# Splitting the second layer's weights piece by piece during the first layer, with a detour through DRAM

## What is computed

```python
def _attn_ref(x, filt_r, filt_i):
    X = np.fft.rfft(x, axis=1)
    F = (filt_r + 1j * filt_i)[None, :, :]
    return np.fft.irfft(X * F, n=x.shape[1], axis=1).astype(np.float32)

def _moe_ref(x, w_in, w_out):                 # first layer
    h = x @ w_in
    g = np.where(h > 0.0, h, np.exp(np.minimum(h, 0.0)) - 1.0)
    return g @ w_out

def _moe2_ref(x, w_in, w_out):                # second layer
    h = x @ w_in
    g = h * np.clip(h + 3.0, 0.0, 6.0) / 6.0
    return g @ w_out
```

## Time and profile before

| | us |
|---|---|
| median of 3 runs | 1116.21 (1115.38 to 1118.57) |
| the profiled execution's own time | 1117.79 |
| its span in the profile | 1116.0 |
| PE busy | 1101.5 (99%) |
| ACT busy | 769.0 (69%) |
| DVE busy | 751.9 (67%) |
| POOL busy | 280.7 (25%) |
| TensorE's mean granted clock | 0.998 of full |

### The profile page before, as it was taken

The page is one execution under the profiler, slowest core; times in us unless marked ns, Lnnn a source line. Parts: engine busy times, 40 slices in busy tenths (PEclk is TensorE's granted clock), DMA queues, the critical chain, the costliest instruction groups (busy, mean ns, idle before and its releaser), DMA issues.

```text
span 1116.0 us, 13377 instructions
## 1 busy us (share of the span) xinstructions
PE 1101.5 (99%) x4796; PEld 882.5 (79%) x4796; DVE 751.9 (67%) x933; ACT 769.0 (69%) x1156; POOL 280.7 (25%) x217
## 2 busy tenths in 40 slices
PE   8999999999999999999999999999999999999998
PEld 4565788888888888888888788888888888888886
DVE  5898566666667666666687866666666665665655
ACT  0445588888788888888899766665666566666654
POOL 3856402102102111111288821111111121120000
PEclk9999999999999999999999999999999999999999
DMA  9665300200200200200311200200101001000000
GB/s 283 195 196 177 132 1 1 75 1 1 74 1 1 75 1 1 75 1 1 112 38 57 93 1 1 75 1 15 61 1 37 37 1 38 37 1 1 38 1 37
DMA packets 29618, 54.98 MB, mean 49 GB/s; under 512 B 3440, under 2 KB 19696, under 8 KB 29552
## 3 DMA queue, kind: packets, MB, share of 16 engines
q1 hardware_dynamic: 22784, 42.98, 11.8%
q10 hardware_dynamic: 6768, 11.16, 2.9%
HBM read 35.61 MB, written 18.51 MB: 48 GB/s over the span
## 4 chain that ended last, share of the span: by engine, by line
PE 85%; ACT 4%; DVE 3%; DMA 3%; POOL 2%; issue 2%; SPq 0%; ACTq 0%; DVEq 0%; POOLq 0%
PE ps L471 43%; PE ps L462 13%; PE ps L461 13%; PE ps L460 13%; DMA w_raw<-w_dev 2%; PE ps L424 2%; DVE e L779 1%; ACT e L626 1%; PE ps L394 1%; ACT e L628 1%; ACT w_hi L598 1%; PE ps L402 1%; DMA x_ring<-x_dev 1%; POOL f_ring L824 1%; PE ps L411 1%
## 5 line engine op out<-in xcount | busy, mean ns | idle before, releaser
L793 DVE TENSOR_TENSOR g_lo<-e,g_hi 128x502 fp32r<-128x502 f32 (+1 forms) x288 | 277.2, 990 | 136.1 <-ACT g_hi L665 135.9
L460 PE MATMUL ps<-op_hi,w_hi 128*128 128x502 f32 x672 | 261.9, 390 | 1.6 <-ACT ps L658 1.6
L462 PE MATMUL ps<-op_lo,w_hi 128*128 128x502 f32 x672 | 261.9, 390 | 0.0
L461 PE MATMUL ps<-op_hi,w_lo 128*128 128x502 f32 x672 | 261.2, 389 | 0.0
L471 PE MATMUL ps<-g_lo,w_hi 128*128 128x502 f32 x766 | 236.8, 390 | 0.8 <-DVE g_lo L793 0.6
L471 PE MATMUL ps<-g_hi,w_hi 128*128 128x502 f32 x766 | 235.6, 389 | 0.0
L471 PE MATMUL ps<-g_hi,w_lo 128*128 128x502 f32 x766 | 234.9, 388 | 0.0
L862 POOL TENSOR_TENSOR op_lo<-op_raw,op_hi 128x1004 fp32r<-128x1004 f32 (+1 forms) x48 | 100.3, 2089 | 488.8 <-ACT op_hi L606 488.8
L471 PEld LDWEIGHTS ps<-g_lo,w_hi 128*128 128x128 f32 x766 | 143.3, 188 | 31.8 <-DVE g_lo L793 3.2
L471 PEld LDWEIGHTS ps<-g_hi,w_lo 128*128 128x128 f32 x766 | 144.1, 188 | 29.3
L471 PEld LDWEIGHTS ps<-g_hi,w_hi 128*128 128x128 f32 x766 | 143.8, 188 | 29.4 <-ACT g_hi L665 0.5
(11 more groups left out here) (73 smaller groups left out, 1154.3 us busy)
## 6 DMA issues: line engine op xcount, KB each, us to landing
op_raw<-y SPq DMA_DIRECT2D x36, 251.0 KB, 3.6
x_ring<-x_dev SPq DMA_DIRECT2D x32, 192.0 KB, 4.6
y<-ystage SPq DMA_DIRECT2D x12, 502.0 KB, 2.9
y<-ystage ACTq DMA_DIRECT2D x24, 235.0 KB, 2.8
out_dev<-ystage SPq DMA_DIRECT2D x11, 502.0 KB, 2.9
f_ring<-f_dev SPq DMA_DIRECT2D x13, 384.0 KB, 3.8
w_raw<-w_dev ACTq DMA_DIRECT2D x16, 256.0 KB, 4.3
w_raw<-w_dev SPq DMA_DIRECT2D x16, 256.0 KB, 3.0
```

The costliest lines, as they stand in the source:

```text
L460: pe.matmul(out, w_hi[p][:, cols], hi, start=start, stop=False, skip_group_check=True)
L461: pe.matmul(out, w_lo[p][:, cols], hi, start=False, stop=False, skip_group_check=True)
L462: pe.matmul(out, w_hi[p][:, cols], lo, start=False, stop=True, skip_group_check=True).then_inc(done, 1)
L793: return dve.tensor_tensor(g_lo[:, tiles, :], e[:, tiles, :], f32(g_hi[:, tiles, :]), ALU.subtract)
```

## The change

The second layer's eight pairs are no longer split at the change of layers, but in super-tiles 1 to 4, two pairs in each: `next_weights(s)` gives pairs 2s - 2 and 2s - 1. Their high and low parts are made in a new SBUF buffer, `w_out`, and stored to a DRAM tensor, `w1_parts`. In super-tile 5, as soon as `d12_done` says that a pair's place is free, SP loads both parts (720,896 bytes each) straight into `w_hi[p]` and `w_lo[p]`.

```diff
+        w1_parts = nc.dram_tensor("w1_parts", (PAIRS, 2, P, WCOL), F32, kind="Internal").ap()
+        w_out = sbuf(ctx, "w_out", [P, 2, WCOL], F32R)
+        def next_weights(s):
+
+            return (2 * s - 2, 2 * s - 1) if 1 <= s <= PAIRS // 2 else ()
...
                 if s:
                     store_out(s - 1, 0)
                     store_out(s - 1, 1)
+                for p in next_weights(s):
+                    load_w(PAIRS + p)
+                for p in next_weights(s):
+                    sp.wait_ge(w_hi_done, PAIRS + p + 1)
+                    sp.dma_start(w1_parts[p, 0], f32(w_out[:, 0, :])).then_inc(w1_hi_stored, 16)
+                    sp.wait_ge(w_lo_done, PAIRS + p + 1)
+                    sp.dma_start(w1_parts[p, 1], f32(w_out[:, 1, :])).then_inc(w1_lo_stored, 16)
                 if s == NS - 1:
+                    sp.wait_ge(w1_hi_stored, 16 * PAIRS)
+                    sp.wait_ge(w1_lo_stored, 16 * PAIRS)
                     for p in range(PAIRS):
-                        load_w(PAIRS + p)
+                        sp.wait_ge(d12_done, (NS - 1) * PAIRS + p + 1)
+                        sp.dma_start(f32(w_hi[p][:]), w1_parts[p, 0]).then_inc(w1_loaded[p], 16)
+                        sp.dma_start(f32(w_lo[p][:]), w1_parts[p, 1]).then_inc(w1_loaded[p], 16)
...
-                    if s % NS == 0:
-                        pe.wait_ge(w_hi_done, s // NS * PAIRS + p + 1)
-                        pe.wait_ge(w_lo_done, s // NS * PAIRS + p + 1)
+                    if s == 0:
+                        pe.wait_ge(w_hi_done, p + 1)
+                        pe.wait_ge(w_lo_done, p + 1)
+                    if s == NS:
+                        pe.wait_ge(w1_loaded[p], 32)
...
-                k = u - 2 - (NS - 1) * PAIRS
-                if 0 <= k < PAIRS:
-                    weight_hi(PAIRS + k)
+                if u < NU and p in (1, PAIRS - 1) and next_weights(s):
+                    weight_hi(PAIRS + next_weights(s)[p // (PAIRS - 1)])
...
-                if s != NS - 1:
-                    for piece in range(NOP if s + 1 < 2 * NS else 0):
-                        operand_lo(s + 1, piece)
-                else:
-                    for k in range(PAIRS):
-                        weight_sums(PAIRS + k)
-                        if 1 <= k <= NOP:
-                            operand_lo(s + 1, k - 1)
-                        weight_lo(PAIRS + k)
+                later = next_weights(s)
+                if later:
+                    weight_sums(PAIRS + later[0])
+                    weight_lo(PAIRS + later[0])
+                for piece in range(NOP if s + 1 < 2 * NS else 0):
+                    operand_lo(s + 1, piece)
+                if later:
+                    weight_sums(PAIRS + later[1])
+                    weight_lo(PAIRS + later[1])
```

More of the change, by code:

```diff
@@ L212, in build @@
         w_sum, w_hi_done, w_lo_done = sem("w_sum"), sem("w_hi_done"), sem("w_lo_done")
+        w1_hi_stored, w1_lo_stored = sem("w1_hi_stored"), sem("w1_lo_stored")
+        w1_loaded = [sem(f"w1_loaded{p}") for p in range(PAIRS)]
         xr_loaded, t_sum = sem("xr_loaded"), sem("t_sum")
@@ L593, in weight_hi @@
             def weight_hi(k):
-                p = k % PAIRS
-                if k >= PAIRS:
-                    act.wait_ge(d12_done, (NS - 1) * PAIRS + p + 1)
+                dst = w_hi[k][:] if k < PAIRS else w_out[:, 0, :]
+                if k > PAIRS:
+                    act.wait_ge(w1_hi_stored, 16 * (k - PAIRS))
+                    act.wait_ge(w_lo_done, k)
                 act.wait_ge(w_sum, 4 * (k + 1))
-                act.copy(w_hi[p][:], w_raw[:, k % 2, P:12 * P]).then_inc(w_hi_done, 1)
+                act.copy(dst, w_raw[:, k % 2, P:12 * P]).then_inc(w_hi_done, 1)
             def operand_hi(s, piece):
@@ L838, in weight_lo @@
             def weight_lo(k):
-                p = k % PAIRS
+                hi, lo = (w_hi[k], w_lo[k]) if k < PAIRS else (w_out[:, 0], w_out[:, 1])
                 pool.wait_ge(w_hi_done, k + 1)
+                if k > PAIRS:
+                    pool.wait_ge(w1_lo_stored, 16 * (k - PAIRS))
                 half = WCOL // 2
[L842 to L845, removed]
+                pool.tensor_tensor(lo[:, 0:half], w_raw[:, k % 2, P:P + half],
+                                   f32(hi[:, 0:half]), ALU.subtract)
+                pool.tensor_tensor(lo[:, half:], w_raw[:, k % 2, P + half:],
+                                   f32(hi[:, half:]), ALU.subtract).then_inc(w_lo_done, 1)
             def operand_sums(s):
```

## The result

| | before | changed kernel |
|---|---|---|
| median, us | 1117.32 (6 runs, 1115.38 to 1118.57) | 1129.37 (6 runs, 1127.09 to 1131.79) |
| span of the profiled execution, us | 1116.0 | 1130.0 |
| the profiled execution's own time, us | 1117.79 | 1131.79 |

The change made the kernel slower by 12 us: the ratio is 1.0106, with a 95% interval of 1.0092 to 1.0121. The changed kernel's runs lie in two groups of three, near 1131 (mean granted clock 0.994 to 0.995 of full) and near 1127.5 (0.996 to 0.998). The profiled execution is of the upper one; a second trace, whose time is that of the lower one, comes with the experiments.

A forecast was written before the change was run, and what follows sets the result against it. PE, busy 99%, was taken to bound the kernel. Waits 20.4, second pair 0.8 and later evacuation 1.8, less 2.5 gained, made 20.5 us more; on the median of 1116.21 the forecast was 1136.7, range 1129 to 1144.

The forecast's parts named there:

- lower bounds: Low end of the sum: four super-tiles at 4.0 us less the 2.5 gained, 13.5 us more, 1129.7.
- What bounds the kernel, and what there was to gain: PE, busy 99%; across the change of layers, removing the splitting of weights gains at most 2.5 us.
- The place of the wait: ACT's weight_hi at p = 1 would wait for POOL's sums of the first pair, in four super-tiles.
- The length of the wait: ACT would stand still 4.9 us at p = 1, making PE's p6 4.0 us late.
- From ACT's wait to p6: 4.42 us from weight_hi's start to the next copy's start, and 0.57 for the copy, before PE's p6.
- The second wait, for g_hi and g_lo: PE's g_lo matmuls in the next iteration would be 5.0 us late, against 4.0 at p6; POOL's low parts hinder DVE.
- The clock rival: TensorE's clock falls in the four new waits, costing 0.7 to 1.7 us each: 1139.5 to 1143.5; chance 32%.
- The second pair at p = 7: Its weight_hi fills ACT's idle time before the evacuation: 0.2 us of PE at each of four boundaries, 0.8.
- The later evacuation: ACT's evacuation some 0.6 us later delays the next group's sums: 0.6 us in super-tiles 2, 3 and 4, so 1.8.
- The stores and the reload: 16 DMAs storing the parts and 16 loads bringing them back, 720,896 bytes each, would cost nothing.
- loads land sooner: Rival: raw weights land at the median 3.1 us, each wait costs 1.7, 6.9 us more: 1123.1; chance 12%.

The follow-up runs named there:

- other pair first: The changed kernel with the two pairs' raw loads in the other order, so the pair needed at p = 1 is loaded second: 1134.99 us.
- the tokens' loads first: The changed kernel with the first pair's weight_hi at p = 2 and the second pair's stores behind the next tokens' loads: 1115.03 and 1115.44 us.
- low part later: The changed kernel with POOL's weight_lo of the first pair moved behind the first operand_lo, weight_hi still at p = 1: 1123.35 us.

## Why the prediction was right, and where its numbers were off

The forecast was 1136.7 us in a range of 1129 to 1144, slower with 95%. The time was 1129.37: the sign and the mechanism were right, the size was not. The forecast increase was 20.5 us, the measured one 12.1, three fifths of it and less than the 13.5 of the lower bounds. That the time lies 0.4 us inside the range is luck: the kernel before came out at 1117.32 over six runs, and on the 1116.21 from which the forecast started the same increase would have given 1128.3.

- **What bounds the kernel, and what there was to gain.** Right. 2.5 us were read from the eight intervals, and 2.48 came; by the second trace of the kernel before it is 1.6.
- **The place of the wait.** Right: ACT at p = 1, four times, for POOL's last sum, in the order of the earlier trace rows.
- **The length of the wait.** This is the step that failed. The prediction put ACT's wait at 4.9 us, and with it 4.0 us before p6 in each super-tile; measured are waits of 2.2 to 2.9 us in one trace and 1.7 to 2.5 in the other, and excesses of 1.8 to 2.6 and 1.3 to 2.1 us. Of the 20.4 us in the sum 16 were this term, and it measured 8.8 and 6.5. "The trace shows this very chain at super-tile 5" took the landing there, 6.5 us, for that of any super-tile. In super-tile 1 it was 224.15 - 219.52 = 4.6. The sums took 2.3 us where they had taken 2.8, and the issue came 0.2 later after ACT's evacuation. 4.9 - 1.9 - 0.5 + 0.2 = 2.7. The row that should have raised a doubt was used for a rival only: a median landing of 3.1. One landing behind other transfers is one value out of a range, here 3.8 to 6.5 us.
- **From ACT's wait to p6.** Right to 0.1 us in super-tile 1: `weight_hi` started at 226.46, and 226.46 + 4.42 + 0.57 = 231.45, PE's p6 at 231.51.
- **The second wait, for g_hi and g_lo.** 1.0 us each was forecast. 0.96 to 1.03 was measured in each of the five cases in which the clock did not fall in these two traces, and moving `weight_lo` took it away. The cause given, DVE's operation beside `weight_lo`, holds together with ACT's lateness, not alone.
- **The clock rival.** It came true in part: three falls in one trace, none behind the waits in the other. The price written was 0.7 to 1.7 each. In the changed kernel it was 0.4 to 0.7 (1.66, 1.63 and 1.41 against 0.96), with the other pair first 0.7 to 1.2. The waits were also shorter than the 4.0 us for which it was weighed.
- **The second pair at p = 7.** 0.8 us were put at the boundaries, and 0.3 came, nearly all of it from u = 41. With the tokens' loads first it was 0, so it is not `weight_hi` at p = 7 that costs it, but the order of tokens and stores on SP, which the prediction had put at nothing.
- **The later evacuation.** 1.8 us were added for it. The evacuation does come later behind p6, 8.6 us in place of 8.2 in super-tiles 2 to 4, but the second raw load is issued 10.49 to 10.53 us behind p6 there and 10.33 in super-tile 1, so that 0.2 us of it are left. No such term is seen in the waits: that of super-tile 4 was the shortest in one trace and that of super-tile 2 in the other.
- **The stores and the reload.** Nothing, as forecast: no wait for `w1_loaded`, and the pace kept from u = 42 on.

The errors went opposite ways. ACT's wait was put at nearly twice its length, 7.2 us too much in the sum, and the clock, left out of the forecast, added 1.7 us in the profiled execution. The "loads land sooner" rival, at 12%, with 6.9 us more was nearer to the measured 12.1 than the forecast's 20.5; the truth lies between the two landings that they took, 3.1 and 6.5 us.

## What to carry to other kernels

Before work is moved ahead of a deadline, look at what it waits for in the new place, not only at whether the engine has room: an in-order engine passes a wait for an operand on to all that stands behind it, here 12 us in four places for a cast of 1.37 us that found room one iteration later. A wait put behind a DMA should be given the slowest and the fastest landing of the trace, and one iteration more if it is free. When an engine feeds the bound engine, place the new instruction by its releaser's time, and then ask what else that instruction sets off (here POOL's subtraction beside DVE's two-input operation, 1.0 us each behind an ACT that was late).

## What was not expected of the hardware

- **The clock and waits of 2 us.** TensorE's granted clock fell to 1.2 GHz for 3.4 us at or soon behind waits before p6 of 1.76, 2.14 and 2.44 us (changed kernel) and 2.12, 2.88 and 2.80 (other pair first). It stayed at 2.4 GHz behind 1.59 (changed kernel), 1.21, 0.94, 1.24 and 1.44 (its second trace), 1.05 to 1.57 (low part later), and also behind 2.54 us (other pair first, super-tile 3). So the length of the wait alone does not decide. A fall costs 0.4 to 1.2 us there, since part of it lies in a wait that would be there anyway.
- **The landing of the same load varies from place to place.** The same 256 KB load behind two stores of 502 KB landed 3.8 to 5.7 us after its issue in most places and 6.2 to 6.5 in one, in both traces of that program, and what decides is open.
- **The filter stage moves by 4 us from run to run.** In the twelve traces the first p6 behind it stands between 134.96 and 138.95 us, though no kernel changes anything there. This is more than all that the change had to gain, so that one execution against another cannot show a gain of 0.2%, while the distance from the first p6 to the last can. Why the stage varies is open.
